# A gate taken by one Silu activation instead of a sigmoid and a product

## The reference, cut to what matters

```python
f = 1.0 / (1.0 + np.exp(-f_logit))
for t in range(S):
    state = f[:, :, t, :, None] * state + einsum(k_t, v_t)
    y[:, :, t] = einsum(q_t, state)
...
g = xn @ w_gate                            # 384 -> 1536
silu = g * (1.0 / (1.0 + np.exp(-g)))
val = xn @ w_val
x = silu * val @ w_out                     # 1536 -> 384
...
h = x @ w_in                               # 384 -> 2048
g = np.where(h >= 1, h, np.where(h <= -1, 0, (h + 1) ** 2 / 4))
return g @ w_out
```

## Time and profile before

| | |
|---|---|
| median of 3 runs | 976.22 us |
| profiled execution | 976.3 us |
| its span, first to last instruction | 974.6 us |
| PE busy | 959.8 us, 98% |
| DVE busy | 573.6 us, 59% |
| ACT busy | 326.1 us, 33% |
| granted TensorE clock | 1.000 of full speed |

### The profile page before, as it was taken

How to read it: one execution, slowest core, us unless ns; L and a number is a source line. 1 busy time by engine, 2 the same in 40 slices (tenths; PEclk the granted TensorE clock), 3 DMA queues, 4 the chain that set the end, 5 groups by cost and what they waited for, 6 DMA issues and landing times.

```text
span 974.6 us, 19135 instructions
## 1 busy us (share of the span) xinstructions
PE 959.8 (98%) x7651; PEld 869.4 (89%) x7651; DVE 573.6 (59%) x1098; ACT 326.1 (33%) x556; POOL 21.0 (2%) x58
## 2 busy tenths in 40 slices
PE   7899999999999999999999999999999999999998
PEld 6899999999999999999999998888888888888886
DVE  8778666565674765665664664545545455445443
ACT  2343322322322222223223443333333343333333
POOL 0000000000000000000000000000000000000000
PEclk9999999999999999999999999999999999999999
DMA  5541111011111120210111310000000000000000
GB/s 195 189 153 43 41 42 50 32 48 40 40 42 39 40 73 8 73 40 22 58 40 50 120 58 1 1 32 0 0 32 0 0 32 0 32 0 0 33 1 33
DMA packets 16766, 42.32 MB, mean 43 GB/s; under 512 B 1376, under 2 KB 7648, under 8 KB 16736
## 3 DMA queue, kind: packets, MB, share of 16 engines
q1 hardware_dynamic: 16736, 41.88, 12.7%
HBM read 37.16 MB, written 4.72 MB: 43 GB/s over the span
## 4 chain that ended last, share of the span: by engine, by line
PE 95%; DVE 3%; issue 1%; ACT 0%; DMA 0%; POOL 0%; DVEq 0%; POOLq 0%
PE gate_ps L417 15%; PE val_ps L417 15%; PE acc L493 13%; PE gate_ps L481 10%; PE val_ps L481 10%; PE acc L439 10%; PE acc L497 7%; PE acc L443 5%; PE tb L328 2%; PE y_ps L352 2%; PE y_ps L358 2%; PE tb L338 1%; DVE qd L739 1%; PE ta L314 1%; DVE after L718 1%
## 5 line engine op out<-in xcount | busy, mean ns | idle before, releaser
L659 ACT ACTIVATE raw<-raw,half_col 128x512 f32<-128x512 f32 x96 | 69.3, 722 | 155.3 <-DVE raw L914 155.3
L493 PE MATMUL acc<-high,low 128*128 128x512 f32 x285 | 110.9, 389 | 0.0
L493 PE MATMUL acc<-high 128*128 128x512 f32 x285 | 110.9, 389 | 0.0
L603 ACT ACTIVATE high<-h_buf 128x384 fp32r<-128x384 f32 x96 | 50.5, 526 | 168.2 <-DVE h_buf L850 168.2
L598 ACT ACTIVATE act_buf<-gate_ps 128x384 f32<-128x384 f32 x96 | 47.2, 492 | 177.1 <-PE gate_ps L417 177.1
L417 PE MATMUL gate_ps<-high 128*128 (+1 forms) x288 | 99.2, 344 | 1.0 <-issue 0.6
L439 PE MATMUL acc<-high 128*128 128x384 f32 x288 | 99.1, 344 | 0.0
L417 PE MATMUL val_ps<-high 128*128 (+1 forms) x288 | 99.1, 344 | 0.0
L417 PE MATMUL gate_ps<-high,low 128*128 (+1 forms) x288 | 96.5, 335 | 0.0
L417 PE MATMUL val_ps<-high,low 128*128 (+1 forms) x288 | 96.4, 335 | 0.0
L417 PE MATMUL gate_ps<-low,high 128*128 (+1 forms) x288 | 96.4, 335 | 0.0
(11 more groups left out here) (120 smaller groups left out, 1906.6 us busy)
## 6 DMA issues: line engine op xcount, KB each, us to landing
raw<-qkf_dram SPq DMA_DIRECT2D x21, 768.0 KB, 4.3
x_all<-wb_dram SPq DMA_DIRECT2D x12, 576.0 KB, 3.9
v_sb<-v_dram SPq DMA_DIRECT2D x24, 192.0 KB, 2.8
out_dram<-x_all SPq DMA_DIRECT2D x5, 768.0 KB, 3.8
raw<-wc_dram SPq DMA_DIRECT2D x7, 384.0 KB, 3.0
x_all<-qkf_dram SPq DMA_DIRECT2D x2, 768.0 KB, 6.0
kd<-wc_dram SPq DMA_DIRECT2D x3, 384.0 KB, 3.2
qd<-wc_dram SPq DMA_DIRECT2D x3, 384.0 KB, 3.4
```

What stands on the lines that cost most here:

```text
L493: pe.matmul(acc[:, m, 0:N2], wc_part(w, j, 1, m), h2_hi[:, j % 2, :], start=(j == 0 and w is w_hi), stop=False)
L659: nc.scalar.activation(act2_buf[:, j % 2, :], act2_buf[:, j % 2, :], ACT.Square, bias=half_col[:, :], scale=0.5).then_inc(square_ready, 1)
```

## The change

ACT's activation of the gate bank is Silu (x times its sigmoid) in place of Sigmoid, and its result in `act_buf` is the whole gated value. DVE's product `use_gate` goes. `use_value` multiplies the value bank with `act_buf`. The activation itself now frees the gate bank (`gate_used`), and before it writes `act_buf` it waits until `use_value` of the step before has read it (`h_ready`). The semaphore between the two old steps goes.

```diff
                 def sigmoid_gate(i, j):
                     act.wait_ge(gate_made, i * JB + j + 1)
-                    act.wait_ge(gate_used, i * JB + j + 1)
-                    nc.scalar.activation(act_buf[:, :], gate_ps[:, 0:N], ACT.Sigmoid).then_inc(sig_ready, 1)
+                    act.wait_ge(h_ready, i * JB + j + 1)
+                    nc.scalar.activation(act_buf[:, :], gate_ps[:, 0:N], ACT.Silu).then_inc(gate_used, 1)
...
-                def use_gate(i, j):
-
-                    dve.wait_ge(sig_ready, i * JB + j + 1)
-                    nc.vector.tensor_tensor(h_buf[:, j % 2, :], gate_ps[:, 0:N], act_buf[:, :], ALU.mult)\
-                        .then_inc(gate_used, 1)
-
                 def use_value(i, j):
                     dve.wait_ge(gate_used, i * JB + j + 2)
                     dve.wait_ge(val_made, i * JB + j + 1)
-                    nc.vector.tensor_tensor(h_buf[:, j % 2, :], val_ps[:, 0:N], h_buf[:, j % 2, :], ALU.mult)\
+                    nc.vector.tensor_tensor(h_buf[:, j % 2, :], val_ps[:, 0:N], act_buf[:, :], ALU.mult)\
                         .then_inc(h_ready, 1)
...
-                        if j == 0:
-                            if split:
-                                split_wb(REST_LATE[0])
-                            use_gate(i, j)
+                        if j == 0 and split:
+                            split_wb(REST_LATE[0])
                         if following is not None:
                             attention(following, 3 * j + 1)
-                        if j > 0:
-                            use_gate(i, j)
```

More of the change, by code:

```diff
@@ L171, in build @@
         gate_made = sem("gate_made")
-        sig_ready = sem("sig_ready")
         gate_used = sem("gate_used")
```

## The result

The changed kernel takes 979.9 us (median of 6 runs, 979.76 to 981.39) against 976.19 us for the kernel before (976.03 to 977.02, 6 runs). The ratio is 1.0039, with a 95% interval of 1.0026 to 1.0052: 0.39% slower. The forecast was 980.3 us.

What follows compares the result with a forecast made beforehand. It took PE, 98% busy, as the bound. Tile 0 +1.38, six boundaries +3.1 and the gate bank -0.5 sum to +4.0 us on the profiled 976.3: 980.3 us, range 977.5 to 985.0.

Steps and rivals of the forecast that it cites:

- The bound, the loads and their size: PE bounds at 98% busy; ACT gets 44 table loads near 1283 ns, reaching 381 us; DVE falls to 520 us.
- Rival 1: At the seven exposed sigmoids a switch also stops ACT ahead of the load: 9.0 us, 989.3 us in all; chance 0.12.
- Most loads are free: On ACT, most of the 55.2 us of added table loads run in waits or behind DVE's queue and cost nothing.
- Silu(1): Gate activation of step 1 in a tile, behind a table load; claimed the tightest covered place, 1.0 us of slack.
- Rival 4: A second place becomes exposed, most likely the load ahead of step 1's Silu: 4.9 us, 985.2 us; chance 0.06.
- Six boundaries, 0.52 us each, +3.1: Starts of tiles 1 to 6: the load delays the first forget-gate sigmoid; 0.52 us each reaches PE's wait for `rest_h`.
- Tile 0, +1.38: First exposed sigmoid of tile 0 moves by 1.38 us, all passed to PE's wait for `rest_h` at 44.01.
- The gate bank, -0.5: Tile 0 at 82.60 us: gate(8) no longer waits for the product of step 7 to free the bank; 0.5 us back.
- the other 95 end nothing that PE waits for: Of the 96 products removed from DVE, all but the one ahead of gate(8) in tile 0 give PE nothing.
- Rival 2: No load reaches PE, being beside the Silu or fewer than the order shows: 975.8 to 976.9 us; chance 0.11.
- rival 3: Faster: 0.55 us freed per step on DVE ends PE's waits for `rest_h` and gate bank: 971.4 us; chance 0.03.

## Why the prediction was right

- **The bound, the loads and their size.** Right: 44 loads of 1283 ns, DVE at 521.7 for 520, ACT at 382.7 for 381. The Trainium skill ("ScalarE: Activation LUTs", section "What ACT_TABLE_LOAD costs") adds a drain of about 1380 ns to a switch. It is in no trace here: sigmoid and Silu start 0.01 to 0.02 us behind a load, and the load as close behind the Silu, wherever neither of them waits for PE. Rival 1 falls by these rows and by the time with it.
- **Most loads are free.** Right, and shown: 29 of them in mid-stream cost 0.2 us together at most. Silu(1), which I took for the tightest with 1.0 us of slack, ended at 254.07 in tile 3, 2.0 us ahead of gate(2). I had measured its slack to the start of the low half before the change, which comes 0.5 us later now and stands 0.5 us ahead of gate(2). Rival 4 had nothing to stand on. Its 985.2 us lay just over the range that was meant to reach it.
- **Six boundaries, 0.52 us each, +3.1.** Right in the sum (3.11) and in the parts: 0.26 us of wait becomes 0.75 to 0.78, and a tile is 0.52 us longer. The product's removal gives nothing here, as forecast, since the kernel with the switch only has the same waits. It gives 0.08 us a boundary only where no load stands in the way, and there an exposed load costs 0.6 us (0.18 to 0.78).
- **Tile 0, +1.38.** It is 1.45. The place was wrong: I had PE wait 3.2 us for `rest_h` at 44.01. PE's value(1) needs h_ready, and I had not asked who waits for `use_value`; so PE stopped there already, for 1.57 us, and its wait for `rest_h` stayed at 1.85. The prediction had named a wait of PE where it had none before as a sign of being wrong, and this is one. The sum did not suffer, since both waits hang on the same chain of DVE, but I had not foreseen that.
- **The gate bank, -0.5.** Too small: 0.87. Gate(8) gave 0.6 for my 0.5. PE also waited for the bank ahead of gate(5), for 0.16 us by the weight load's row (as the rows of the kernel with the switch only show), right behind a wait for `rest_h`. That gave 0.2, and I had looked at the larger wait alone: "the other 95 end nothing that PE waits for" was wrong by one product.
- **Rival 2 and rival 3.** The first is out by the two kernels with exposed and covered loads only. The third had its mechanism half right: the product's removal is worth 1.4 us with no exposed load and 0.9 with them, and not 4.9.

The errors of the three terms are +0.1 (tile 0), -0.4 (gate bank) and nothing (boundaries), and 980.3 came out as 979.9.

## What to carry to other kernels

An activation of another table set costs a load where the functions change, not where the new one stands: list the loads in ACT's order, and ask of each whether the engine waits for something at that place anyway. Where one has no cover, move the odd function to where the engines wait, here ahead of the gate's activation. One load then ran in ACT's wait and the other in DVE's, and the kernel that had become 0.4% slower was 0.2% faster than before, and 0.5% with one more reorder (971.57 us). A step that gives little or nothing in one version (the low half first, 0.8 us) can give 2.6 us in another, when the second wait behind it, here for a bank, is gone.

## What the runs showed that I had not expected

- PE's clock fell after a single gap in an otherwise full stream: 3.01 us of idle by the weight loads' row (2.7 by the matmuls') and then about 3.4 us at 1.2 GHz, from between 0.5 us ahead of the gap's end and 1.5 us behind it, while 1.57 us and then 1.85 us of idle (1.25 and 1.53 by the matmuls) with work between them, in the changed kernel at 39 to 46 us, left it at 1.00. With it 7 x 3.00 = 21.0 us of delay became 24.8.
- Four activations of 128x1, 203 ns for one alone, take 0.48 us in a row behind another activation, and hold back what follows by 0.38 us.
